# Linear-attention pairs of heads beside two feed-forward layers on one core: inversion earlier in VectorE's order, the key exponential of pair 0 later, one key tile between the query products, and the last tokens' part of the key sums added by VectorE

## The reference

```python
def phi(x):
    proj = x @ w_phi                                   # 64 -> 128 features
    proj = proj - max(abs(proj), axis=-1, keepdims=True)
    return concatenate([exp(proj), exp(-proj)], axis=-1)
q_p, k_p = phi(q), phi(k)
kv = einsum('bhsf,bhsd->bhfd', k_p, v)
z = sum(k_p, axis=2)
num = einsum('bhsf,bhfd->bhsd', q_p, kv)
den = einsum('bhsf,bhf->bhs', q_p, z) + 1e-06
x = num / den                                          # attention's output
# first layer: xk, xr mix x with the token before; r = sigmoid(xr @ w_r)
x = r * (relu(xk @ w_k) ** 2 @ w_v)
# second layer: h = relu(x @ w_in); gate = sigmoid(conv of 3 tokens(h)); out = (h * gate) @ w_out
```

## Time and profile before

| | |
|---|---|
| time, three runs | 1274.17, 1275.68, 1275.94 us (median 1275.68) |
| profiled execution, its own time | 1277.55 us |
| its span, first to last instruction | 1275.7 us |
| mean granted clock of TensorE | 0.997 of full |
| busy PE, DVE, ACT, POOL | 98%, 68%, 45%, 11% of the span |
| chain that ended last | PE 83%, DVE 8%, DMA 3%, issue 3%, ACT 2% |

### The profile page before, as it was taken

One profiled execution on the slowest core, in us unless ns is written; L12 is line 12 of the kernel. 1 busy time (PEld: TensorE's weight loads), 2 busy tenths in 40 slices (PEclk: granted clock), 3 DMA queues, 4 the chain that ended last, 5 costly groups with the idle time before them and its releaser, 6 DMA issues.

```text
span 1275.7 us, 23373 instructions
## 1 busy us (share of the span) xinstructions
PE 1252.8 (98%) x9332; PEld 1095.9 (86%) x9332; DVE 865.8 (68%) x1372; ACT 577.1 (45%) x1049; POOL 142.8 (11%) x137
## 2 busy tenths in 40 slices
PE   8899999999999999999999999999999999999998
PEld 6678798888888879889888888999889899898997
DVE  7789677667667866767667776647585593673863
ACT  4553634625535463463543654455344352352441
POOL 3412111202111211121111211000000000000000
PEclk9999999999999999999999999999999999999999
DMA  5512221221212212222122121421102102012001
GB/s 175 162 43 62 65 59 54 66 68 40 72 58 60 68 51 59 63 67 59 48 82 59 41 79 29 139 67 51 70 1 79 51 21 79 1 71 79 1 34 42
DMA packets 88243, 78.89 MB, mean 62 GB/s; under 512 B 58440, under 2 KB 67016, under 8 KB 87112
## 3 DMA queue, kind: packets, MB, share of 16 engines
q1 hardware_dynamic: 87976, 77.33, 19.9%
q10 hardware_dynamic: 160, 0.07, 0.0%
HBM read 58.21 MB, written 19.01 MB: 61 GB/s over the span
## 4 chain that ended last, share of the span: by engine, by line
PE 83%; DVE 8%; DMA 3%; issue 3%; ACT 2%; SPq 0%; POOL 0%; DVEq 0%; ACTq 0%
PE psm L610 32%; PE ps L610 18%; PE psh L1292 6%; PE psh L1293 6%; PE psh L1291 6%; PE pso L1293 5%; PE pso L1292 5%; PE pso L1291 5%; DMA den<-den_scr 2%; DMA den_scr<-den_cols 1%; DVE k_max L1025 1%; DVE mix L1111 1%; DVE q_part L1035 1%; DVE q_turn L1032 1%; PE ps L718 1%
## 5 line engine op out<-in xcount | busy, mean ns | idle before, releaser
L610 PE MATMUL psm<-xy_hi,wk_hi 128*128 128x288 f32 x512 | 156.3, 305 | 4.5 <-ACT relu L940 3.3
L610 PE MATMUL psm<-k_hi,wv_hi 128*128 128x288 f32 x512 | 154.5, 302 | 0.0
L610 PE MATMUL psm<-k_lo,wv_hi 128*128 128x288 f32 x512 | 151.6, 296 | 0.0
L610 PE MATMUL psm<-k_hi,wv_lo 128*128 128x288 f32 x512 | 151.5, 296 | 0.0
L1293 PE MATMUL psh<-xy_hi,win_lo 128*128 128x288 f32 x512 | 151.3, 296 | 0.0
L1291 PE MATMUL psh<-xy_hi,win_hi 128*128 128x288 f32 x512 | 151.3, 296 | 0.0
L1292 PE MATMUL psh<-xy_lo,win_hi 128*128 128x288 f32 x512 | 151.3, 296 | 0.0
L610 PE MATMUL psm<-xy_lo,wk_hi 128*128 128x288 f32 x512 | 151.1, 295 | 0.0
L610 PE MATMUL psm<-xy_hi,wk_lo 128*128 128x288 f32 x512 | 150.7, 294 | 0.0
L598 POOL TENSOR_TENSOR z_pairs<-k_signs 128x512 f32<-128x512 f32 x56 | 73.0, 1303 | 596.1 <-ACT k_signs L873 592.1
L873 ACT ACTIVATE k_signs<-k_signs 128x1152 f32<-128x1152 f32 x32 | 37.2, 1164 | 170.7 <-DVE k_signs L1027 156.2
(11 more groups left out here) (159 smaller groups left out, 2825.9 us busy)
## 6 DMA issues: line engine op xcount, KB each, us to landing
k_in<-in_k SPq DMA_DIRECT2D x32, 320.0 KB, 3.3
v_nat<-in_v SPq DMA_DIRECT2D x32, 320.0 KB, 3.5
q_in<-in_q SPq DMA_DIRECT2D x32, 288.0 KB, 3.0
y_scr<-y SPq DMA_DIRECT2D x64, 144.0 KB, 1.8
y<-y_scr SPq DMA_DIRECT2D x8, 1152.0 KB, 5.8
den<-den_scr SPq DMA_DIRECT2D x60, 144.0 KB, 3.0
out<-rows SPq DMA_DIRECT2D x32, 256.0 KB, 2.1
stage<-in_moe_w_in SPq DMA_DIRECT2D x4, 512.0 KB, 3.7
```

The lines of the kernel that those rows point to most:

```text
L610: return nc.tensor.matmul(o, lhsT, rhs, start=first, stop=last, skip_group_check=True)
```

## The change

Four edits. RC moves from behind QT to behind E. EL of pair 0 moves behind the first layer's second full tile (K+ 0 1) in all batches, as it stood in the first one. In E, head 1's key tile 0 is issued between the query products, and the rest keep their order, one tile of head 1 ahead. In KV, the products of the ones with the last tokens' tile go; a new step ZA behind each M lets VectorE add that tile to z_tiles, 64 partitions for each head, and TensorE waits for it (z_added) before its products with z_tiles.

```diff
--- before.py
+++ after.py
@@ -85,14 +85,16 @@
 
 
 BESIDE_NEXT = {
-    ("M", 0): [("XK", 1, 0)],
-    ("QT", 1): [("RC", 0)],
-    ("M", 1): [("HK", 1, 0), ("LK", 1, 0)] + mixing("K", 1, 1) + [("XR", 1, 0)],
+    ("K+", 0, 1): [("EL", 0)],
+    ("M", 0): [("ZA", 0), ("XK", 1, 0)],
+    ("E", 1): [("RC", 0)],
+    ("M", 1): [("ZA", 1), ("HK", 1, 0), ("LK", 1, 0)] + mixing("K", 1, 1) + [("XR", 1, 0)],
     ("WQ", 1): [("HR", 1, 0), ("LR", 1, 0)] + mixing("R", 1, 1) + [("DV", 0)],
-    ("QT", 2): [("RC", 1)],
+    ("E", 2): [("RC", 1)],
     ("PICK", 2): [("DV", 1)],
-    ("QT", 3): [("RC", 2)],
-    ("M", 3): [("DV", 2), ("XK", 2, 0), ("HK", 2, 0)],
+    ("E", 3): [("RC", 2)],
+    ("M", 2): [("ZA", 2)],
+    ("M", 3): [("ZA", 3), ("DV", 2), ("XK", 2, 0), ("HK", 2, 0)],
     ("WQ", 3): [("LK", 2, 0), ("XR", 2, 0)],
     ("R", 1, 3): [("HR", 2, 0), ("LR", 2, 0)],
     ("V-", 1, 0): [("RC", 3)],
@@ -101,11 +103,10 @@
 BESIDE_SECOND = {
     **BESIDE_NEXT,
     ("K+", 0, 0): [("EK", 0)],
-    ("K+", 0, 1): [("EL", 0)],
-    ("M", 0): mixing("R", 0, 0) + mixing("R", 0, 1),
+    ("M", 0): [("ZA", 0)] + mixing("R", 0, 0) + mixing("R", 0, 1),
     ("PICK", 0): [("D1", WIDE)],
     ("NUM", 0): [("D1", WIDE + 1)],
-    ("QT", 1): [("XK", 1, 0), ("RC", 0)],
+    ("QT", 1): [("XK", 1, 0)],
 }
 BESIDE_LAST_PAIR = {**BESIDE_NEXT, ("V", 1, 1): [], ("V", 1, 2): [("DV", 3)] + mixing("K", 2, 1)}
 ALONE = {
@@ -147,7 +148,7 @@
         for step in attention_steps():
             if step == ("E", 0) and batch == 0:
                 out += [("D0", PAIRS - 1)] + mixing("K", 0, 1)
-            elif step not in (("EK", 0), ("EL", 0)) or batch:
+            elif step not in (("EK", 0), ("EL", 0)) or step[0] == "EK" and batch:
                 emit(step)
             fill(FILL_NS.get(step[0], 0))
     for u, t in enumerate(tiles):
@@ -333,8 +334,8 @@
     k_max_ready, k_tail_shifted, k_shifted = sem("k_max_ready"), sem("k_tail_shifted"), sem("k_shifted")
     k_exp_ready = sem("k_exp_ready")
     kv_summed, kvz_copied = sem("kv_summed"), sem("kvz_copied")
-    z_paired, z_presummed, kvt_copied, kv_turned, z_copied = (
-        sem("z_paired"), sem("z_presummed"), sem("kvt_copied"), sem("kv_turned"), sem("z_copied"))
+    z_paired, z_presummed, z_added, kvt_copied, kv_turned, z_copied = (
+        sem("z_paired"), sem("z_presummed"), sem("z_added"), sem("kvt_copied"), sem("kv_turned"), sem("z_copied"))
     features, q_exp_ready = sem("features"), sem("q_exp_ready")
     z_weighted, q_weighted, num_summed, den_copied = sem("z_weighted"), sem("q_weighted"), sem("num_summed"), sem("den_copied")
     first_den, first_inverse, x_half, exp_loaded = sem("first_den"), sem("first_inverse"), sem("x_half"), sem("exp_loaded")
@@ -624,13 +625,15 @@
             own, cols = slice(D * h, D * h + D), slice(*CHUNKS[h][chunk])
             return mm(q_cols(h, p, a)[:, cols], phi[own, :], q_in[own, p % 2, cols], first, False)
 
-        def project_queries(p, a):
+        def project_queries(p, a, first_key=False):
 
             mm(k_tail(p, a), k_in[:, p % 2, P * (TT - 1):P * TT], phi[:], True, True).then_inc(shared_bank, 1)
             feature_chunk(p, a, 1, 1, True)
             feature_chunk(p, a, 0, 1, True).then_inc(shared_bank, 1)
             await_(pe, shared_bank, 2 * PAIRS, a, 2 * p + 1)
             feature_chunk(p, a, 0, 0, True)
+            if first_key:
+                key_tile(p, 1, 0)
             await_(pe, shared_bank, 2 * PAIRS, a, 2 * p + 2)
             feature_chunk(p, a, 1, 0, False).then_inc(raw_features, 1)
 
@@ -641,10 +644,11 @@
             await_(pe, z_copied, PAIRS, a - 1, p)
             await_(pe, q_loaded[p % 2], 16 * (PAIRS // 2), a, 16 * (p // 2 + 1))
             await_(pe, k_loaded[p % 2], 16 * (PAIRS // 2), a, 16 * (p // 2 + 1))
-            project_queries(p, a)
+            project_queries(p, a, first_key=True)
             for t in range(TT - 1):
-                for h in (0, 1):
-                    last = key_tile(p, h, t)
+                last = key_tile(p, 0, t)
+                if t + 1 < TT - 1:
+                    last = key_tile(p, 1, t + 1)
             last.then_inc(k_projected, 1)
 
         def features_only(p, a):
@@ -703,13 +707,11 @@
                 for h in range(2):
                     tile = KEYS - 1 if t == TT - 1 else (TT - 1) * h + t
                     mm(sums_turned()[D * h:D * h + D, 0:2, :], v_nat[:, t, h, 0:D], k_signs[:, :, tile, :], t == 0, t == TT - 1)
-            pe.wait_ge(z_presummed, 2 * PAIRS * (a - 1) + 2 * p + 2)
-            for t in (0, TT - 1):
-                for h in range(2):
-                    for e in range(2):
-                        row = 32 * (2 * h + e)
-                        last = mm(sums_turned()[row:row + 1, 2, :], v_nat[:, t, h, D:D + 1],
-                                  k_signs[:, e, KEYS - 1, :] if t else z_tiles[:, e, h, :], t == 0, t == TT - 1)
+            pe.wait_ge(z_added, 2 * PAIRS * (a - 1) + 2 * p + 2)
+            for h in range(2):
+                for e in range(2):
+                    row = 32 * (2 * h + e)
+                    last = mm(sums_turned()[row:row + 1, 2, :], v_nat[:, 0, h, D:D + 1], z_tiles[:, e, h, :], True, True)
             last.then_inc(kv_summed, 1)
 
         def turn_back(p, a):
@@ -1059,6 +1061,14 @@
                 nc.vector.scalar_tensor_tensor(out=weighted_q[:, h, :], in0=q_exp[:, 1, h, :], scalar=kvz[:, 1, h, D:D + 1],
                                                in1=weighted_q[:, h, :], op0=ALU.mult, op1=ALU.add).then_inc(q_weighted, 1)
 
+        def add_last_tokens(p, a):
+
+            dve.wait_ge(z_presummed, 2 * PAIRS * (a - 1) + 2 * p + 2)
+            dve.wait_ge(k_exp_ready, 2 * PAIRS * a + 2 * p + 2)
+            for h in range(2):
+                own = slice(D * h, D * h + TAIL)
+                nc.vector.tensor_tensor(z_tiles[own, :, h, :], z_tiles[own, :, h, :], k_signs[own, :, KEYS - 1, :], ALU.add).then_inc(z_added, 1)
+
         def invert(p, a):
             dve.wait_ge(den_spread, spread(p, a) + (16 if weighted(p, a) else 32))
             await_(dve, inverse_stored, 16, sent(p, a), 0)
@@ -1159,6 +1169,8 @@
                     spread_maxima(step[1], a)
                 elif kind == "WQ" and weighted(step[1], a):
                     weigh_q(step[1], a)
+                elif kind == "ZA":
+                    add_last_tokens(step[1], a)
                 elif kind == "RC":
                     invert(step[1], a)
                 elif kind in ("D0", "D1"):
```

## The result

The changed kernel takes 1263.38 us (median of 4 runs, 1262.14 to 1264.32), the one before 1274.93 (median of 4): a ratio of 0.9911, 95% interval 0.9894 to 0.9929. On another chip the same two gave 0.9920 (0.9897 to 0.9943). The profiled execution took 1263.98 us, its span is 1262.2; before it was 1277.55 and 1275.7. Forecast were 1266.3 us and a gain of 11.2 us between the profiles. It is 13.5.

A forecast was written before the change was run, and what follows sets the result against it. TensorE, busy 98% of the span, was taken as the bound. Terms -6.0 + 6.3 + 1.9 - 3.7 + 2.4 - 7.1 - 5.0 = -11.2 us took 1277.55 to 1266.3, range 1260 to 1272 for 8 in 10.

The forecast's parts named there:

- What bounds it: Whole kernel: TensorE, busy for 98% of the span; the end moves only if it gets less work or waits less.
- Row products: KV: four products of the last tokens go from each of 28 pairs, 0.216 us each pair, -6.0 us.
- Key tile: Step E: one of head 1's key tiles moved among the query products saves 0.18 us a pair, -5.0 us.
- The bound from the idle time: Step E: a tile moved into the 0.33 us idle in head 1's row half shortens the end by 0.22.
- Exponential: Pair 0: EL behind two tiles ends the fourth tile's wait for the relu, five times 0.51 and once 1.17, -3.7 us.
- Pair 0's new wait: Pair 0, product on z_tiles: later max_blocks leaves 0.45 us where the additions need 0.83; 6 x 0.4 = +2.4 us.
- Pair 3's new wait: Pair 3, before the product on z_tiles: TensorE waits for the additions, 7 x 0.9 = +6.3 us.
- The bound of 0.4: Pair 3: lower bound, 0.4 us per batch, on TensorE's wait for the additions; the upper was 1.05.
- The forecast 0.83 us: From the end of max_blocks until TensorE sees the additions complete: 0.78 us, and 0.05 more.
- The sharing with GpSimd: VectorE and GpSimd share an SBUF port; whichever starts first holds it for its whole instruction. Nothing in the sum hangs on it.
- First batch: First batch with GpSimd's sums: PICK's old wait now stands behind the additions and product; with pair 0's 0.6, +1.9 us.
- Inversion: RC starts about 3.5 us sooner, so DV2 in pair 3 no longer waits for its DMA: -7.1 us, slow clock included.

## Why the prediction was right, point by point

- *What bounds it.* TensorE, at 98% before and after; each edit's effect is found in TensorE's starts alone.
- *Row products.* -0.216 a pair: shown by pairs 1 and 2, 22.33 with the key tile alone and 22.11 with the additions as well.
- *Key tile.* 0.22 a pair, not 0.18: -6.2 us for -5.0. The bound from the idle time was the value.
- *Exponential.* 0.61 a pair for 0.51, 4.3 us for 3.7.
- *Pair 0's new wait.* The products with z_tiles stand 14.81 us behind the mark with the additions and 14.34 without: 0.47 for 0.4. Alone, the additions find 1.39 us of room there and cost nothing; the wait arises only where they meet the later EL.
- *Pair 3's new wait.* 13.61 against 12.82, 0.79 for 0.9. The bound of 0.4 was too hopeful. I gave the sooner inversion 0.1 us on max_blocks; it gave 0.24 (12.99 us behind the mark with the inversion alone, 13.23 before). The forecast 0.83 us from max_blocks to TensorE came out, by luck in part: the two additions start 0.44 us apart, not 0.35, but the first starts 0.08 before max_blocks has ended. The sharing with GpSimd went as described: the copy of q_part started 0.40 us before z_tiles ended and ended with it, a k_lo got ahead of z_pairs, and z_pairs took 1.43 us for its 1.29 (VectorE's copy and k_lo, then GpSimd's z_tiles and z_pairs, changed kernel):

```profile
352.37 0.45 DVE L1041 COPY q_part<-q_part 128x64 f32<-128x64 f32 x1
...
352.75 2.82 DVE L1145 TENSOR_TENSOR k_lo<-square,k_hi 128x288 fp32r<-128x288 f32 x3
...
352.03 0.74 POOL L602 TENSOR_TENSOR z_tiles<-z_pairs 128x256 f32<-128x256 f32 x1
...
352.92 1.43 POOL L599 TENSOR_TENSOR z_pairs<-k_signs 128x512 f32<-128x512 f32 x1
```

- *First batch.* Its first two stretches are 55.22 and 55.57 in two profiles and 54.22 without additions. With the 0.43 that the products give, that is a wait of 1.4 and 1.8 for 1.9.
- *Inversion.* All 7.1 us of excess went, slow clock included, and -6.6 was measured alone. The sum holds because it priced the additions' wait with the inversion already moved. But -7.1 is the lateness of one profile, not a fixed worth of the move: with the additions in place the move is worth 2.9 to 3.2 us between the profiles, 1.7 of them by a shorter wait for the additions and 1.0 by the one late inverse. And the prediction put all lateness to the load being issued late. In one of its three slow batches the load was issued as early as usual and landed late (below).

Alone, the four edits save 21 us by their medians (6.6, 4.9, 6.9 and 2.6), together 11.5. By the parts in the table it is 25.0 and 13.5. Of that difference of 11.5 about 10 is lateness counted more than once: the single edits' pair 3 sums have 7.0, 2.3, 1.6 and 6.2 us less of it than the kernel before, 17.1 in all, and only 7.0 could go. Pair 0's wait, which no single edit has, is 2.8, and the shorter wait for the additions gives 1.6 back.

The terms as measured: -6.0 - 6.2 - 4.3 - 7.1 + 5.5 + 2.8 + 1.4 = -13.9, for 13.5 between the profiles. By them the forecast missed 2.7 us: 1.2 in the key tile, 0.8 in pair 3's wait, 0.6 in the exponential, 0.5 in the first batch, less 0.4 in pair 0.

Why the inverse is late at times can be read from the traces, too. The store to den_scr is followed by the load as soon as it has landed. SP's issues of two batches of the kernel before, and two lines of its page on DMA queues (packets, MB, share of 16 engines):

```profile
251.60 0.33 SPq L502 DMA_DIRECT2D den_scr<-den_cols  x1
...
255.01 1.12 SPq L509 DMA_DIRECT2D den<-den_scr  x2
...
464.53 0.33 SPq L502 DMA_DIRECT2D den_scr<-den_cols  x1
...
465.95 1.12 SPq L509 DMA_DIRECT2D den<-den_scr  x2
...
q8 instruction: 75, 1.23, 0.4%
q14 instruction: 32, 0.26, 0.1%
```

The load comes 3.4 us after the store in the first batch. In the second it comes the usual 1.4 us after, but needs 4.8 us to land, where 3.5 to 3.8 is usual. The traces have the single DMA packets. The first store is 144 packets; 135 of them start by 252.62, the last nine only between 253.95 and 254.06, and a packet of 16 KB of the queue called instruction ran from 252.57 to 253.97. The store of the next batch's pair 3 shows the same: such a packet from 360.13 to 361.49, and the last nine of 144 from 361.48 on. In the batch of 464.53 such a packet ran from 468.34 to 469.40, while the loads were under way.

Over the 13 profiles, four to eight of the 30 stores per run have their load more than 1.8 us behind them, 76 in all, half of them near the same times of the run (34 to 50, 245 to 252, 354 to 371). Ahead of 55 us they fall among the large first loads. Of the 53 later ones, 47 had an instruction packet under way before the store landed, of the 311 other stores 10. Of the 31 loads that took over 4.3 us, all had one, of the 333 others 98. No run moved these packets, so this rests on the traces alone; they leave little else. Whether pair 3's inverse meets such a packet depends on all that comes before it. Therefore the single edits' medians can't be split to better than a microsecond or two, while the stretches without a DMA in them repeat to 0.02 us.

## What to carry to other kernels

Read a change to a TensorE-bound kernel as marks on TensorE's timeline, pair by pair: work moved to an idle engine is free only in the places where TensorE comes later than that work ends, and it may be kept for those places alone (here pairs 1 and 2, worth 6 to 8 us over the change as made). Before adding up the terms of several edits, ask whether two of them wait at the same place: a new wait ahead of an old one covers part of it, and moving the old one's cause then gains less. A term for waits that come and go (a late DMA here) is worth what the profile at hand happened to have; compare it with more than one profile. In row-tiled stages, look at the two halves of the array apart; the idle time in one of them is room for a product that is on the other's way.

## What the runs showed of the hardware that was not expected

- Products for one row half started 0.16 us before an earlier instruction's last pass in the other half (300.67 and 300.83).
- Short additions on VectorE overlap only in part. The two of 64 x 256, one per head, last 0.41 and 0.42 us, and the second starts 0.03 behind the first one's end. Of the four of 64 x 128 (0.28 us each) the two of one head start 0.20 us apart, and the change to the other head's partitions again has 0.03 us between end and start.
- Storing 4.5 KB to DRAM takes 1.4 us as a rule from its issue to the next load's, and up to 4.25 at times; the two loads that bring it back, repeated over the partitions, take 3.3 to 5.5 us more. One 16 KB packet of instructions, 1.4 us long, held up nine of the store's 144 packets.
- After 2.5 us of TensorE idle time the granted clock was at 1.2 GHz for 3.5 us; after waits of 1.6 and 0.9 us in the other batches, and of 2.1 and 2.2 us in the run with the key tile alone, it stayed at 2.4 GHz.
